# PV in two runs of three key tiles a unit, and PSUM dealt out anew, in an attention and two-layer-MLP kernel

## The reference, cut to what matters

```python
q_assign = np.argmax(np.einsum('bhsd,hcd->bhsc', q_n, c_n), axis=-1)
k_assign = np.argmax(np.einsum('bhsd,hcd->bhsc', k_n, c_n), axis=-1)
mask = q_assign[:, :, :, None] == k_assign[:, :, None, :]
scores = np.where(mask, scale * np.matmul(q, k.transpose(0, 1, 3, 2)), -1000000000.0)
attn = np.exp(scores - np.max(scores, axis=-1, keepdims=True))
attn = attn / (np.sum(attn, axis=-1, keepdims=True) + 1e-09)
attn_out = np.matmul(attn, v)
...
h = (x @ w1) * (x @ w2) @ w3;  x = h @ w_out
h = x @ w_in;  out = (h * np.clip(h + 3.0, 0.0, 6.0) / 6.0) @ w_out2
```

## Time and profile before

| what | value |
|---|---|
| median of 3 runs | 719.99 us (719.34 to 720.17) |
| the profiled execution | 720.99 us, of which its span is 719.2 us |
| PE busy | 711.0 us, 99% of the span |
| PEld, DVE, ACT, POOL busy | 600.8, 473.6, 415.4, 447.6 us |
| chain of work that ended last | PE 94%, DVE 3%, ACT 1%, DMA 1% |
| granted TensorE clock | 1.0 of full speed throughout |

### The profile page before, as it was taken

One profiled execution on the slowest core, in us unless ns is written; L12 is line 12 of the kernel. 1 busy time (PEld: TensorE's weight loads), 2 busy tenths in 40 slices (PEclk: granted clock), 3 DMA queues, 4 the chain that ended last, 5 costly groups with the idle time before them and its releaser, 6 DMA issues.

```text
span 719.2 us, 11817 instructions
## 1 busy us (share of the span) xinstructions
PE 711.0 (99%) x4017; PEld 600.8 (84%) x4017; DVE 473.6 (66%) x706; ACT 415.4 (58%) x856; POOL 447.6 (62%) x455
## 2 busy tenths in 40 slices
PE   8999999999999999999999999999999999999998
PEld 6777666666666666999999999999988889998886
DVE  5237667666766684677986778978856547885221
ACT  6317676767676785444545545477754448774333
POOL 5954454443444465896979978877646759853321
PEclk9999999999999999999999999999999999999999
DMA  8648867867667411221001210012211223221112
GB/s 294 183 105 227 151 129 141 181 118 152 149 146 140 112 18 45 81 75 58 1 31 60 89 60 0 30 60 74 74 59 60 73 102 125 83 74 57 65 41 88
DMA packets 41771, 68.49 MB, mean 95 GB/s; under 512 B 10224, under 2 KB 17904, under 8 KB 41712
## 3 DMA queue, kind: packets, MB, share of 16 engines
q1 hardware_dynamic: 40128, 64.85, 35.2%
q10 hardware_dynamic: 1584, 2.88, 1.0%
HBM read 44.07 MB, written 3.19 MB: 66 GB/s over the span
## 4 chain that ended last, share of the span: by engine, by line
PE 94%; DVE 3%; ACT 1%; DMA 1%; SPq 0%; issue 0%; POOL 0%; ACTq 0%
PE ps L1312 21%; PE ps L1313 21%; PE ps L1314 21%; PE ps L1437 10%; PE ps L1423 8%; PE ps L1411 6%; PE ps L1413 5%; PE ps L1381 1%; DVE g_lo L1230 1%; DMA wo_raw<-in_wo 1%; PE ps L1398 1%; PE ps L1390 1%; DVE sum_lo L1131 1%; DVE x_lo L1147 0%; PE ps L1343 0%; PE ps L1346 0%
## 5 line engine op out<-in xcount | busy, mean ns | idle before, releaser
L620 POOL TENSOR_TENSOR b_lo<-stage,b_hi 128x512 fp32r<-128x512 f32 x94 | 112.5, 1198 | 102.8 <-ACT b_hi L860 101.0
L1230 DVE TENSOR_TENSOR g_lo<-gate,g_hi 128x384 fp32r<-128x384 f32 x96 | 83.9, 882 | 65.0 <-ACT g_hi L922 64.9
L1110 DVE TENSOR_REDUCE neg_max<-ps 128x1 f32<-128x768 f32 x96 | 91.6, 954 | 44.5 <-PE ps L1413 44.5
L922 ACT CAST g_hi<-gate 128x384 fp32r<-128x384 f32 x96 | 49.2, 514 | 91.0 <-PE ps L1314 91.0
L777 ACT ACTIVATE probs<-ps,neg_max 128x768 f32<-128x768 f32 x96 | 86.8, 904 | 14.5 <-DVE neg_max L1110 13.0
L1423 PE MATMUL ps<-ident,probs 128*128 128x128 f32 x576 | 78.8, 272 | 0.6 <-ACT probs_t L877 0.6
L877 ACT COPY probs_t<-ps 128x512 f32<-128x512 f32 x96 | 54.4, 585 | 38.4 <-PE ps L1423 38.0
L1437 PE MATMUL ps<-probs_t,v_raw 128*64 128x384 f32 x384 | 75.4, 502 | 0.0
L1131 DVE TENSOR_TENSOR sum_lo<-sum_raw,sum_hi 128x768 fp32r<-128x768 f32 x64 | 65.3, 1023 | 14.7 <-ACT sum_hi L836 14.4
L1314 PE MATMUL ps<-b_hi,g_lo 128*128 128x512 f32 x192 | 74.8, 389 | 0.0
L1313 PE MATMUL ps<-b_lo,g_hi 128*128 128x512 f32 x192 | 74.8, 389 | 0.0
(11 more groups left out here) (129 smaller groups left out, 1847.1 us busy)
## 6 DMA issues: line engine op xcount, KB each, us to landing
stage<-in_wio SPq DMA_DIRECT2D x64, 256.0 KB, 2.6
qk_ops<-qk_split SPq DMA_DIRECT2D x32, 384.0 KB, 5.4
stage<-in_w SPq DMA_DIRECT2D x46, 256.0 KB, 3.2
qk_raw<-in_qk SPq DMA_DIRECT2D x16, 384.0 KB, 7.0
qk_ops<-qk_split SPq DMA_DIRECT2D x32, 192.0 KB, 4.8
v_raw<-in_v SPq DMA_DIRECT2D x16, 192.0 KB, 3.2
recip_all<-recip_rows SPq DMA_DIRECT2D x32, 96.0 KB, 3.0
out<-out_sb ACTq DMA_DIRECT2D x11, 256.0 KB, 2.2
```

What stands on the lines that cost most here:

```text
L620: nc.gpsimd.tensor_tensor(b_lo[n % 2][:, cols], stage[n % 2][:, cols], b_hi[n % 2][:, cols].bitcast(F32), ALU.subtract).then_inc(s_lo[half ...
L1110: nc.vector.tensor_reduce(neg_max[:, g:g + 1], scores[g % 2], AX.X, ALU.max, negate=True).then_inc(s_max, 1)
L1230: nc.vector.tensor_tensor(g_lo[i][:], hidden(q, c, f)[0][:], g_hi[i][:].bitcast(F32), ALU.subtract).then_inc(s_glo, 1)
```

## The change

PSUM has eight banks. Before, each `scores` tile lay across two banks as 512 + 256 columns, the ring had two banks and PV had two. Now a `scores` tile has a half row (384 columns) in each of two banks, so that the four banks 0 to 3 hold half rows; the ring has three banks (4, 5, 6), and PV has one (7). A score's two matmuls of a half follow each other, and `row_max` and `exp` read two pieces of 384. PV of a unit, before in four runs of 1, 1, 2 and 2 key tiles, now runs as tiles 0 to 2 at the start of step 2 and as tiles 3 to 5 at the end of step 4. With one bank for it, PV of unit u waits for `x_normed(u-1)`, before for `x_normed(u-2)`. In steps 2, 3 and 4 the transposes come ahead of the score. The steps of preparing a head are given out anew (`ahead`), L and H now together in step 2, H two steps later than before; on DVE `x_normed`, `best_rank` and `reciprocals` now stand ahead of the row maximum of step 0. SP's order is as it was.

```diff
-RING_BANKS, PV_BANKS = (4, 5), (6, 7)
+RING_BANKS, PV_BANK = (4, 5, 6), 7
-DVE_GROUPS = (0, 2, 7)
-PV_STEPS = {0: (4, 5), 2: (1,), 4: (2, 3)}
+DVE_GROUPS = (1, 3, 5)
...
-def prepared(s):
-    n, step = divmod(s + AHEAD, ST)
-    return (n + 2 if n + 2 < HEADS else None), step
+def ahead(s, by):
+    n = s // ST + by
+    return n if n < HEADS else None
...
-        scores = [ps[:, 2 * i:2 * i + 2, :].rearrange("p a b -> p (a b)")[:, 0:S] for i in range(2)]
+        scores = [ps[:, 2 * i:2 * i + 2, 0:HALF] for i in range(2)]
...
+                for half in range(2):
+                    tile, cols = scores[s % 2][:, half, :], slice(half * HALF, (half + 1) * HALF)
+                    nc.tensor.matmul(tile, ops[:, 0, q], ops[:, 2, cols], start=True, stop=False)
+                    mm = nc.tensor.matmul(tile, ops[0:MASK_ROWS, 1, q], ops[0:MASK_ROWS, 3, cols], start=False, stop=True)
...
-                    if unit >= 2:
-                        pe.wait_ge(s_xr, unit - 1)
+                    if unit >= 1:
+                        pe.wait_ge(s_xr, unit)
...
+                if s % ST == 0 and s >= 2 * ST:
+                    x_normed(s // ST - 2)
+                if s % ST == 0 and s >= ST and ahead(s, 2):
+                    best_rank(ahead(s, 2))
+                if s % ST == 0 and s >= ST:
+                    reciprocals(s // ST - 1)
...
+                unit, step = s // ST - 1, s % ST
+                if step == 2 and unit >= 0:
+                    for t in range(ST // 2):
+                        p_times_v(unit, t)
+                transposes_first = step in (2, 3, 4)
...
+                if step == 4 and unit >= 0:
+                    for t in range(ST // 2, ST):
+                        p_times_v(unit, t)
+                if step == 2 and ahead(s, 3):
+                    logits(ahead(s, 3))
+                if step == 2 and ahead(s, 2):
+                    hot(ahead(s, 2))
+                if step == 5 and ahead(s, 3):
+                    logit_columns(ahead(s, 3))
```

More of the change, by code:

```diff
@@ L67, in ring_order @@
             uses += [("probs", unit * GROUPS + j // GROUP) for j in range(ST * i, ST * i + ST) if j % GROUP == 0]
-        n, step = prepared(s)
-        if n is not None and step in (1, 3, 5):
-            uses.append((("logits", "cols", "hot")[step // 2], n))
+        if s % ST == 2 and ahead(s, 3):
+            uses.append(("logits", ahead(s, 3)))
+        if s % ST == 2 and ahead(s, 2):
+            uses.append(("hot", ahead(s, 2)))
+        if s % ST == 5 and ahead(s, 3):
+            uses.append(("cols", ahead(s, 3)))
     return uses
@@ L708, in _ @@
                     last_weight_sum(GATE0)
+                if s % ST == 0 and s >= ST and ahead(s, 2):
+                    hot_columns(ahead(s, 2))
                 if s % ST == 0 and s >= 2 * ST:
                     x_low(s // ST - 2)
[L711 to L721, removed]
+                if s % ST == 1 and ahead(s, 3):
+                    scale_q(ahead(s, 3))
+                    split_hi(ahead(s, 3))
+                if s % ST == 4 and ahead(s, 3):
+                    split_lo(ahead(s, 3), 0)
+                    split_lo(ahead(s, 3), 1)
             for q in range(4):
@@ L887, in _ @@
                     block_high_next(GATE0 + 1, 0)
-                if n is not None and step == 5:
-                    mask_rows(n)
                 if s % ST == 0 and s >= 2 * ST:
                     x_high(s // ST - 2)
+                if s % ST == 2 and ahead(s, 3):
+                    rows_of_logits(ahead(s, 3))
+                if s % ST == 2 and ahead(s, 2):
+                    mask_rows(ahead(s, 2))
             def copy_out(g, k):
@@ L1174, in _ @@
             for s in range(SLOTS + 1):
[L1175 to L1179, removed]
+                if s % ST == 0 and s >= 2 * ST:
+                    x_normed(s // ST - 2)
+                if s % ST == 0 and s >= ST and ahead(s, 2):
+                    best_rank(ahead(s, 2))
+                if s % ST == 0 and s >= ST:
+                    reciprocals(s // ST - 1)
+                groups_first = s % ST >= 2
+                if groups_first:
                     group_copies(s)
@@ L1195, in _ @@
                     sums_low(GATE0, True)
-                if n is not None and step_of == 3:
-                    best_of(n)
+                if s % ST == 5 and ahead(s, 3):
+                    best_of(ahead(s, 3))
             def sum_quarter(g, which):
@@ L1408, in score @@
                     pe.wait_ge(s_exp, s - 1)
[L1409 to L1413, removed]
+                ops, q = qk_ops[n % 3], slice(i * P, (i + 1) * P)
+                for half in range(2):
+                    tile, cols = scores[s % 2][:, half, :], slice(half * HALF, (half + 1) * HALF)
+                    nc.tensor.matmul(tile, ops[:, 0, q], ops[:, 2, cols], start=True, stop=False)
+                    mm = nc.tensor.matmul(tile, ops[0:MASK_ROWS, 1, q], ops[0:MASK_ROWS, 3, cols], start=False, stop=True)
                 mm.then_inc(s_scores, 1)
@@ L1461, in _ @@
             for s in range(SLOTS + 1):
[L1462 to L1464 removed]
+                unit, step = s // ST - 1, s % ST
[3 more added lines that the diff above has]
+                transposes_first = step in (2, 3, 4)
+                if transposes_first:
+                    transposes(s - 1)
                 if s + 2 < SLOTS:
@@ L1468, in _ @@
                     fold(7, 6, 8)
-                if s >= 1:
+                if s >= 1 and not transposes_first:
                     transposes(s - 1)
[L1471 to L1476, removed]
+                if step == 4 and unit >= 0:
[7 more added lines that the diff above has]
+                    logit_columns(ahead(s, 3))
             def wide_product(g, k):
```

50 lines of the change are left out of this document (24 added, 26 removed).

## The result

The changed kernel takes 722.86 us (median of 13 runs, 721.21 to 725.62) against 720.66 (13 runs, 719.34 to 721.57): a ratio of 1.0035, interval 1.0022 to 1.0047. It is slower by 0.35%; the prediction had said 716.0, within 710.5 to 721.0.

A forecast was written before the change was run, and what follows sets the result against it. It took PE, almost always busy in attention, as the bound. PE's saving of -9.8 us, +4.2 from SP's queue and +1.6 from short steps made -4.0, so a median of 716.0 us, range 710.5 to 721.

The forecast's parts named there:

- What comes back: the queue of SP: SP's queue lands reciprocals late for x_normed: 0.7 us of PE stall at each of six odd heads, +4.2 us (0 to 9).
- The loop takes all: Rival, chance 0.15: loop from mask_rows over landing and x_normed back takes 14.0 us a unit, above 13.75; 724 us.
- Even heads: load_ops waits for no score; reciprocals 0.4 us late or less beyond the slack, counted within the 0.13 a unit.
- the short steps: PE's steps 5, 0 and 1, with no PV between: waits of 0.13 us a unit, +1.6 us (0 to 3.6).
- What stands behind x_normed: DVE and ACT work up to the copy freeing a bank for T behind H: about 5.5 us, slack 0.6.
- sign of being wrong: A unit above 14.3 us, runs of three over 2.2 us, or the MLP part moving more than 1 us.
- PE's own work: PE's instructions in attention: 0.54 us less a unit, 6.5 over twelve; with both ends -9.8 us (-8 to -11.5).
- the start: Attention's first stretch: most of PE's idle 1.6 us at L, C and H goes, 1.0 us saved (0 to 1.6).
- The price of leaving the full width: PE leaving the array's full width: 0.10 us on each side outside a run, besides 0.15 in it.
- The halves: Score products of 384 + 384 columns instead of 512 + 256: -0.04 us a unit (0 to -0.18).
- The queue is on time: Rival, chance 0.20: masks issued later find emptier rings, PE stays packed, -9.8 and about 0.8 back, 711 us.
- The runs save less: Rival, chance 0.10: PV next to scores or two-bank reads cost more, PE's gain halves to 5; 719.5 us.

The follow-up runs named there:

- with ACT's queue: Changed kernel with the reciprocals' store and spread issued from ACT's DMA queue instead of SP's (SP keeps the last unit's): 714.33 us, ratio 0.9913 to the kernel before.
- both orders: Changed kernel with scale_q ahead of hot_columns on POOL and the reciprocals' spread ahead of the masks on SP: 734.73 us, ratio 1.0193 to the kernel before.

## Why the prediction was wrong

**The step that failed** is the one that sized what comes back, under "What comes back: the queue of SP". It found the late landing, and its numbers were near: `x_normed` at 170.14 comes 16.1 us behind the issue of `load_ops` at 154.07, against 15.15 taken and 16.0 as the upper row. It also named the ring, as its second rival, "The loop takes all", from `mask_rows` over the landing to `mask_rows`, with 14.0 us a turn and 724 us as the time. That is what happened, and the forecast gave it 0.15. From what PE saved in the trace, 9.4 us came back (spans of 712.4 us with ACT's queue and 721.8 without), where this term had 4.2. Three things were mis-sized:

- *Even heads.* The prediction took them to be "0.4 late or less beyond the slack", and had no stall for them but a share of its 0.13 a unit for the short steps. A ring does not know odd and even: DVE waited in all 13 units from 82.73 to 257.46, 16.3 us, mean 1.25, and not in six.
- *What stands behind x_normed.* It followed DVE to the copy that frees a bank for "T behind H" and so allowed a slack of 0.6. The path that counted goes through POOL, where `scale_q` had been put behind `hot_columns` and `x_low`, to L ahead of those transposes; and at the PV bank PE waited 2.1 us in 5 times. Its turn of 14.0 had 6.1 us from `x_normed` to `mask_rows`; the trace has 6.5 to the first mask issue, and the masks to the landing 8.5 and 9.0 (161.60 to 170.14, 176.63 to 185.68) where it took 7.9.
- *The ring as a ring.* A late landing was priced as a delay against a fixed demand and added up over six heads. In a ring the delay is not paid once: each turn starts where the last one ended. The unit is no shorter than the longer of PE's 13.98 and the ring's turn.

Between PV's first run of unit 0 and of unit 12 are 168.16 us with ACT's queue (68.27 to 236.43) and 175.63 in the changed kernel (69.12 to 244.75), against 171.76 before. The ring thus costs 7.5 us there, where the prediction had 4.2. A unit takes 14.64 us, above the 14.3 that the prediction gave as its sign of being wrong.

**PE's own work** was right in kind and nearly in size. With ACT's queue, where PE is full, the span is 712.4 against 719.2, -6.8, where -9.8 and the +1.6 for the short steps make -8.2. By parts: the start -2.0 (-1.0 predicted); twelve units -3.6 (-6.5 and +1.6, -4.9); the last part -1.8 (-2.3); the MLP part +0.6 (0). What the 2.0 at the start come from is open: the change also moves a bank of the fold (`FOLD`) and adds a wait ahead of the first score, which no run undoes. A unit saves 0.32 (14.30 to 13.98) and loses some 0.15 to the short steps, so PE's own saving is some 0.47 where the prediction had 0.54. The run of three was right (2.09 against 2.07). The price of leaving the full width, "0.10 on each side" and 0.15 in the run, fits too: with ACT's queue there are 4.37 us from the transposes at 88.40 to those at 92.77, and a pair (1.36), a score (0.71) and three tiles (1.92) leave 0.38, where the prices give 0.35. The halves gave nothing, where 0.04 had been taken. The Trainium skill's drain ("TensorE: Matmul & The Clock Gate", Part 2: some 128 cycles, 0.053 us), which the prediction weighed as the price of a mode change, makes the merge an estimated 0.16 us a unit; the runs show more than twice that, and the measurement decides.

**The short steps** are nearly as predicted: with ACT's queue the pair of transposes and score at 80.31 takes 1.56 us to 81.87, and the same pair a unit later 1.48 (94.34 to 95.82), where others take 1.36. That is 0.12 to 0.20 a unit against 0.13.

**The rivals.** "The queue is on time" said 711; the kernel in which it is on time has 714.3, 6.5 us below the kernel before beside it, where the rival had 9.0. "The loop takes all" was right in place and within 1.1 us in time, the latter in part by luck: it had 12 us for the ring and 9.8 for PE's saving, both above the 9.4 and the 6.8 (with the short steps) of the traces, and the two errors partly cancel. "The runs save less" was not borne out: it halved PE's saving, and a unit kept 0.47 of 0.54.

## What to carry to other kernels

When work is taken from the engine that bounds a loop, draw every ring of dependences that closes in one turn of the loop, the DMA queue's order included, and compare its length with the new turn: the turn is no shorter than the longer of the two, and slack that once hid the ring is the first thing that the saving eats. A transfer that waits its turn in one engine's queue behind others that wait for late work is part of that ring; another engine's queue can cut it. And the edits of such a change are to be tried in pairs: the merge cost 10 us by itself, gave nothing with its new order, and saved 11 with one queue moved.

## What the runs showed of the hardware

The clock can fall inside a loop in which PE is busy for 158.00 of 170 us (70 to 240). In the kernel with the spread ahead of the masks PE stood still for 2.87 us ahead of 84.04; the stretches around it (columns as in the earlier trace rows, the granted clock third from the end) and the PV run in it:

```profile
81.00:84.00 3.00, 0.17 (x2) 0.00 (x0) 2.39 (x6) 1.81 (x4) 1.39 (x3) 1.00 0.10 23
84.00:86.00 2.00, 1.96 (x12) 1.66 (x14) 0.96 (x1) 1.00 (x3) 1.96 (x3) 0.85 0.94 186
86.00:88.00 2.00, 2.00 (x8) 0.71 (x6) 0.00 (x0) 1.52 (x4) 1.96 (x2) 0.50 1.03 241
88.00:90.00 2.00, 2.00 (x13) 0.93 (x9) 0.15 (x1) 0.00 (x0) 0.10 (x1) 0.80 0.94 175
```

```profile
85.69 3.68 PE L1439 MATMUL ps<-probs_t,v_raw 128*64 128x384 f32 x12
```

The run took 3.68 us, not 2.16, at a granted clock of 0.50, the lower level of 1.2 GHz. The wait of 2.87 us so cost 4.4. Of this kernel's seven waits for the masks, the clock fell to 0.50 behind three (2.87 us, 1.83 at 145.10, 2.25 at 177.07) and stayed at 1.00 behind four (1.54 at 115.24, 1.93 at 208.62, 1.58 at 238.23, 1.63 at 267.13); with both orders it stayed so behind one of 2.40 at 145.16. So the length of the wait does not decide by itself, and what else does is not shown. The three slower runs (3.68, 3.85 and 2.86 us) make 3.9 of that kernel's 10 us.
